# RWKV heads, a dense gated layer and routed experts: per-head products on quarters of TensorE, and a new order ahead of the dense stage

## The reference

```python
# 1: 4 sequences, 8 heads, 768 steps, 48 wide
for t in range(S):
    kt, vt, rt = k[:, :, t], v[:, :, t], r[:, :, t]
    cur = einsum('bhd,bhe->bhde', u[None] * kt, vt)
    y[:, :, t] = einsum('bhd,bhde->bhe', rt, state + cur)
    state = w[None, :, :, None] * state + einsum('bhd,bhe->bhde', kt, vt)
# 2: x (3072, 384), ff 1536
x = (silu(x @ w_gate) * (x @ w_val)) @ w_out
# 3: 8 experts, ff 1024, the best one per token
logits = x @ w_gate2;  e = argmax(logits);  gate = softmax(logits)[e]
out = gate * sigmoid(x @ w_output_gate)[e] * (relu(x @ w1[e]) @ w2[e])
```

## Time and profile before

| | us |
|---|---|
| Runs | 886.81, 887.0, 889.1 (median 887.0) |
| Profiled execution | 887.55 |
| its span | 885.7 |
| TensorE busy | 851.0 |
| VectorE busy | 570.2 |
| ScalarE, POOL busy | 316.5, 182.4 |
| First dense matmul starts | 44.65 |

### The profile page before, as it was taken

The page is one execution under the profiler, slowest core; times in us unless marked ns, Lnnn a source line. Parts: engine busy times, 40 slices in busy tenths (PEclk is TensorE's granted clock), DMA queues, the critical chain, the costliest instruction groups (busy, mean ns, idle before and its releaser), DMA issues.

```text
span 885.7 us, 15606 instructions
## 1 busy us (share of the span) xinstructions
PE 851.0 (96%) x5725; PEld 759.2 (86%) x5725; DVE 570.2 (64%) x1045; ACT 316.5 (36%) x503; POOL 182.4 (21%) x145
## 2 busy tenths in 40 slices
PE   5799999999999999999999999999699999999996
PEld 4688888888888888888888888899699999999995
DVE  8778756675568546543444446467778778977771
ACT  1233223111311131112211221356176766777661
POOL 4923202232123403140101001003112111011110
PEclk9999999999999999999999999999799999999999
DMA  9843420242024402340010002547397778766700
GB/s 380 285 162 132 132 105 13 83 153 83 0 64 128 135 1 65 100 130 1 11 45 36 1 1 80 208 180 238 144 415 258 260 278 302 263 237 252 286 17 19
DMA packets 35935, 125.79 MB, mean 142 GB/s; under 512 B 4044, under 2 KB 19328, under 8 KB 30256
## 3 DMA queue, kind: packets, MB, share of 16 engines
q1 hardware_dynamic: 31504, 108.20, 34.4%
q0 software_dynamic: 3520, 9.87, 2.9%
q10 hardware_dynamic: 864, 7.08, 2.2%
HBM read 107.32 MB, written 18.88 MB: 142 GB/s over the span
## 4 chain that ended last, share of the span: by engine, by line
PE 91%; DVE 3%; DMA 3%; issue 2%; POOL 1%; ACT 0%; POOLq 0%; DVEq 0%
PE bank L1525 33%; PE bank L1569 6%; PE bank L1571 6%; PE bank L1570 6%; PE bank L1622 4%; PE bank L1620 4%; PE bank L1621 4%; PE bank L1601 4%; PE bank L1602 3%; PE bank L1603 3%; PE bank L1598 3%; PE bank L1450 3%; PE bank L1470 2%; PE bank L1435 2%; PE bank L1462 2%
## 5 line engine op out<-in xcount | busy, mean ns | idle before, releaser
L1525 PE MATMUL bank<-X1H,WH 128*128 128x512 f32 x432 | 169.5, 392 | 4.2 <-DVE X1L L1040 4.2
L1525 PE MATMUL bank<-X1H,WL 128*128 128x512 f32 x432 | 168.9, 391 | 0.0
L1525 PE MATMUL bank<-X1L,WH 128*128 128x512 f32 x432 | 168.7, 390 | 0.0
L1186 DVE TENSOR_TENSOR TT<-bank,SG 128x512 f32<-128x512 f32 x72 | 49.7, 691 | 120.5 <-ACT SG L764 120.0
L764 ACT ACTIVATE SG<-bank 128x512 f32<-128x512 f32 x72 | 43.0, 598 | 234.6 <-PE bank L1525 229.9
L694 ACT ACTIVATE AH<-PP 128x512 fp32r<-128x512 f32 (+1 forms) x78 | 46.2, 599 | 162.3 <-DVE PP L1191 162.3
L1525 PEld LDWEIGHTS bank<-X1H,WH 128*128 128x128 f32 x432 | 81.5, 189 | 21.1 <-issue 4.3
L1525 PEld LDWEIGHTS bank<-X1H,WL 128*128 128x128 f32 x432 | 81.4, 188 | 17.1
L1194 DVE TENSOR_TENSOR AL<-PP,AH 128x512 fp32r<-128x512 f32 (+1 forms) x78 | 63.2, 817 | 50.9 <-ACT AH L694 49.4
L1525 PEld LDWEIGHTS bank<-X1L,WH 128*128 128x128 f32 x432 | 81.6, 189 | 16.7
L1569 PE MATMUL bank<-AH,WH 128*128 128x512 f32 (+1 forms) x234 | 91.0, 389 | 0.0
(11 more groups left out here) (225 smaller groups left out, 1859.6 us busy)
## 6 DMA issues: line engine op xcount, KB each, us to landing
W_EVEN<-w SPq DMA_DIRECT2D x20, 1536.0 KB, 9.1
W_ODD<-w SPq DMA_DIRECT2D x18, 1536.0 KB, 7.7
RK_IN<-unit_rk SPq DMA_DIRECT2D x18, 736.0 KB, 5.6
V_IN<-unit_v SPq DMA_DIRECT2D x18, 448.0 KB, 3.8
STG<-w_dense ACTq DMA_DIRECT2D x6, 1152.0 KB, 5.9
X<-mixed SPq DMA_DIRECT2D x6, 768.0 KB, 4.4
mixed<-YS SPq DMA_DIRECT2D x40, 96.0 KB, 2.0
XG_ODD<-store SPq DMA_DIRECT2D x9, 394.0 KB, 8.5
```

The lines of the kernel that those rows point to most:

```text
L1186: tt(TT[:, :], GATE_PS[:, :], SG[:, :], ALU.mult).then_inc(gate_free, 1)
L1525: last = mm(bank_[:, :], lhs[:, f, m, k * P:k * P + P], rhs[:, k, :], start=(x == 0), stop=(x == len(terms) - 1))
```

## The change

Key sums and the state's part of the outputs are made per head: SELU and ST lose the empty halves (64 and 48 columns in place of 112), and each head's product takes 48 rows and up to 64 columns on one quarter of the array. Heads are placed so that the row half and the column half of a head are chosen apart (class `Head`: x rows, g columns, s place among the keys). Products of the two row halves go to two banks: outputs to banks 5 and 6, key sums to 7 and 0, the gate's bank; units 0 to 5 keep one bank for their key sums and make them in two parts. `own_key` and `add_output` read two banks with two instructions each, state decay and state addition take one instruction in place of two. `scores` and the masked part keep their counts of products. Routing uses the gate's bank, except at its last time, and stands ahead of the unit's pieces.

In the head the decays come in a transfer of their own; SELU is one copy; TensorE turns the identity 30 times first; POOL starts behind the power tables; VectorE scales k and r of unit 4 too and takes all six slices of the first weights' low part; X1 is stored, loaded and split in four parts of 128 tokens; units 6 and 7 are loaded behind X1; outputs and state terms of unit 5 move into step 0 of block 0. The diff, cut:

```diff
+HEAD_AT = ((0, 1, 2, 3), (5, 4, 7, 6))
+HALF_COLS = PAIRS * P // 2
+class Head:
+    def __init__(self, h):
+        self.h, self.j, self.g = h, h // 2, h % 2
+        self.x = 0 if h in HEAD_AT[0] else 1
+        self.s = HEAD_AT[self.x].index(h)
+        self.rows = slice(64 * self.x, 64 * self.x + HD)
+        self.out = 64 * self.g
+        self.keys = slice(self.s * P, self.s * P + P)
+        self.cols = slice(self.j * P, self.j * P + P)
+BY_QUARTER = [Head(h) for h in (0, 5, 1, 4, 2, 7, 3, 6)]
...
+    SELU = place(a, "SELU", [PR, PAIRS, 64])
+    ST = place(a, "ST", [PR, BATCH, PAIRS, HD])
...
-                self.scores = bank[5], bank[6]
-                self.c_bank, self.y, self.u = bank[7], bank[5], bank[6]
+                self.scores = self.y = bank[5], bank[6]
+                self.c_banks, self.u = (bank[7], bank[0]), bank[7]
...
         def _(sp):
-            sp.dma_start(CST[:, :], consts).then_inc(consts_loaded, 16)
+            sp.dma_start(CST[:, C_W:C_ID], consts[:, C_W:C_ID]).then_inc(decays_loaded, 16)
+            sp.dma_start(CST[:, C_ID:C_ALL], consts[:, C_ID:C_ALL]).then_inc(consts_loaded, 16)
...
+            def load_x1_part(b):
+                sp.wait_ge(y_start_stored[b], 32)
+                sp.dma_start(X1[:, :, b * P:b * P + P], mixed_tiles[:, :, b * P:b * P + P]).then_inc(x1_part_loaded[b], 16)
             store_output(Unit(0, 0))
+            store_output(Unit(0, 1))
+            load_x1_part(0)
+            load_x1_part(1)
+            store_output(Unit(0, 2))
+            store_output(Unit(0, 3))
+            load_x1_part(2)
+            load_x1_part(3)
             load_unit(Unit(1, 2))
             load_unit(Unit(1, 3))
-            for b in range(1, BATCH):
-                store_output(Unit(0, b))
-            sp.wait_ge(y_start_stored, 32 * BATCH)
-            sp.dma_start(X1[:, :, :], mixed_tiles[:, :, 0:BLK]).then_inc(x1_loaded, 16)
...
         def _(pool):
+            pool.wait_ge(pow_turned, 1)
             scale_rk(u0)
             scale_rk(u1)
+            pool.wait_ge(r_start_scaled, 3)
             pool.wait_ge(tables_ready, 1)
...
-            first_low(0)
             scale_rk(u4)
-            scale_k(u4)
-            scale_r(u4)
             scale_rk(u5)
+            pool.wait_ge(r_start_scaled, 5)
             scale_k(u5)
             scale_r(u5)
             scale_kt(u4)
             scale_kt(u5)
-            first_low(1)
+            pool.wait_ge(x1_low, KT)
...
         def _(act):
+            for b in range(BATCH):
+                first_state(b)
+            x1_high_part(0)
+            x1_high_part(1)
             split_dense(0)
-            first_state(2)
-            first_state(3)
+            x1_high_part(2)
+            x1_high_part(3)
...
         def _(dve):
-            dve.wait_ge(consts_loaded, 16)
+            dve.wait_ge(decays_loaded, 16)
+            nc.vector.tensor_copy(SELU[:, :, :], ucol.unsqueeze(2).broadcast_to([PR, PAIRS, 64])).then_inc(select_ready, 1)
...
-                tt(u.ys, u.v[0:PR, I_VT:I_VV], u.c_bank[0:PR, :], ALU.mult).then_inc(c_used, 1)
+                for x in range(2):
+                    cols = slice(HALF_COLS * x, HALF_COLS * (x + 1))
+                    last = tt(u.ys[:, cols], u.v[0:PR, I_VT:I_VV][:, cols], u.c_banks[x][0:PR, cols], ALU.mult)
+                last.then_inc(c_used, 1)
...
-                    tt(old, old, WPOW[r:r + HD, :, 7:8].broadcast_to([HD, PAIRS, HD]), ALU.mult).then_inc(decayed, 1)
+                tt(ST[:, u.b, :, :], ST[:, u.b, :, :], WPOW[:, :, 7:8].broadcast_to([PR, PAIRS, HD]), ALU.mult)\
+                    .then_inc(decayed, 1)
...
+            mask_scores(u0)
+            dve.wait_ge(pow_turned, 2)
+            mask_scores(u1)
+            first_scales(u2)
+            own_key(u0)
+            add_output(u0)
+            own_key(u1)
+            add_output(u1)
+            first_scales(u3)
+            mask_scores(u2)
+            own_key(u2)
+            mask_scores(u3)
+            own_key(u3)
+            add_output(u2)
+            add_output(u3)
+            first_scales(u4)
+            dense_lows(0, (0,))
+            x1_low_part(0)
+            x1_low_part(1)
+            mask_scores(u4)
+            own_key(u4)
+            x1_low_part(2)
+            x1_low_part(3)
+            finish_unit(u4)
+            dense_lows(0, (1, 2))
+            mask_scores(u5)
+            own_key(u5)
...
         def _(pe):
+            def key_sums(u, quarters=BY_QUARTER):
...
-                for j in range(PAIRS):
-                    last = mm(u.c_bank[0:PR, j * P:j * P + P], SELU[:, j, :], u.rxk[:, j * P:j * P + P],
+                for a in quarters:
+                    width = HD if a.g else 64
+                    last = mm(u.c_banks[a.x][a.out:a.out + width, a.cols], SELU[a.rows, a.s, 0:width], u.rxk[a.rows, a.keys],
                               start=True, stop=True)
...
-                    for j in range(PAIRS):
-                        mm(u.y[0:PR, j * P:j * P + P], ST[:, u.b, j, :], u.rw[:, j * P:j * P + P],
-                           start=(j == 0), stop=False, skip_group_check=True)
+                    for a in BY_QUARTER:
+                        mm(u.y[a.x][a.out:a.out + HD, a.cols], ST[a.rows, u.b, a.s, :], u.rw[a.rows, a.keys],
+                           start=(a.j % 2 == 0), stop=False, skip_group_check=True)
...
+            for x in range(30):
+                nc.tensor.transpose(bank[2][:, 0:P], ident, ident)
+            scores(u0)
+            scores(u1)
...
             outputs(u4)
             state_terms(u4)
-            outputs(u5)
-            state_terms(u5)
+            key_sums(u5, STRAIGHT)
+            scores(u5)
+            key_sums(u5, CROSSED)
...
             def dense_block(n):
+                    if f % 2 == 1 and f // 2 < len(units):
+                        pe.wait_ge(c_used, units[f // 2].i + 1)
                     up(GATE_PS, 0, f, n).then_inc(gate_ready, 1)
                     need(pe, value_free, q)
                     up(VALUE_PS, 1, f, n).then_inc(value_ready, 1)
+                    if not first and f in (0, 1, 2, 3, 5):
+                        if f == 0:
+                            turn(n)
...
+                    if first and f == 0:
+                        outputs(u5)
+                        state_terms(u5)
                     if f // 2 < len(units):
                         u = units[f // 2]
                         if f % 2 == 0:
+                            pe.wait_ge(gate_free, q + 1)
                             key_sums(u)
                             scores(u)
```

More of the change, by code:

```diff
@@ L247, in __init__ @@
             self.odd = b % 2
+            self.behind = self.i - 1 if isinstance(c, int) and self.i == AHEAD else self.i
             self.start = isinstance(c, int) and self.i < AHEAD
@@ L1436, in key_sums @@
                               start=True, stop=True)
-                last.then_inc(c_ready, 1)
+                if quarters[-1].h == 6:
+                    last.then_inc(c_ready, 1)
+                else:
+                    last.then_inc(straight_sums, 1)
+            STRAIGHT = [a for a in BY_QUARTER if a.x == a.g]
+            CROSSED = [a for a in BY_QUARTER if a.x != a.g]
             def scores(u):
-                pe.wait_ge(k_start_scaled if u.first else k_scaled, u.i + 1)
-                pe.wait_ge(r_start_scaled if u.first else r_scaled, u.i + 1)
+                by_dve = u.start and u.i <= BATCH
+                pe.wait_ge(k_start_scaled if by_dve else k_scaled, u.i + 1)
+                pe.wait_ge(r_start_scaled if by_dve else r_scaled, u.i + 1)
@@ L1442, in scores @@
                 if u.start:
                     need(pe, masked, 2 * u.i - 2 if u.i >= 2 else 0)
+                    need(pe, y_added, BATCH if u.i == AHEAD - 1 else 0)
                 else:
-                    pe.wait_ge(y_added, u.i)
-                    pe.wait_ge(state_ready, min(u.i, UNITS - BATCH) if isinstance(u.i, int) else u.i)
-                for j in range(PAIRS):
-                    for half in range(2):
-                        r = 64 * half
-                        last = mm(u.scores[half][:, j * P:j * P + P], u.kw[r:r + HD, j * P:j * P + P],
-                                  u.rw[r:r + HD, j * P:j * P + P], start=True, stop=True)
-                        if j == PAIRS - 1:
+                    pe.wait_ge(y_added, u.behind)
@@ L1453, in scores @@
+                for s in range(PAIRS):
+                    for x in range(2):
+                        a = Head(HEAD_AT[x][s])
+                        last = mm(u.scores[x][:, a.keys], u.kw[a.rows, a.keys], u.rw[a.rows, a.keys], start=True, stop=True)
+                        if s == PAIRS - 1:
                             last.then_inc(scores_ready, 1)
@@ L1475, in state_terms @@
                 pe.wait_ge(kt_scaled, u.i + 1)
-                if u.start:
-                    need(pe, state_ready, min(u.i, BATCH))
-                for j in range(PAIRS):
```

(11 more changed lines are left out.)

317 lines of the change are left out of this document (151 added, 166 removed).

## The result

Four runs after: 878.01 to 880.20 us, median 879.37. Four before, shared with them: 886.81 to 889.1, median 887.99. The ratio is 0.9899 with an interval of 0.9879 to 0.9919: 8.6 us less, and the interval leaves no doubt that it is faster. The forecast of 876.0 was 3.4 us too low and its range held. The quarters brought about what was forecast for them; the new head brought almost nothing.

A forecast was written before the change was run, and what follows sets the result against it. TensorE, 91% of the chain, was taken as the bound. Terms -9.0 + 1.6 + 0.3 - 6.7 - 1.6 + 2.1 + 2.0 = -11.3 took the profiled 887.55 to 876.2, stated as 876.0 us, range 870 to 883.

The forecast's parts named there:

- (c): First step of blocks 1 to 4: TensorE stands still 0.4 us for own_key beside POOL's product, 1.6 us for four.
- (d): Block 5: turning logits and counting ranks in bank 0, with a wait behind each, costs 0.3 us.
- first dense matmul: End of the head: the first dense matmul starts near 37.9 instead of 44.65, 6.7 us less (36 to 41).
- first 18 dense matmuls at full clock: Start of the dense stage: 18 matmuls take 4.1 instead of 5.81 us, 1.6 less if TensorE comes busy.
- unit 5's outputs in block 0: Outputs and state terms of unit 5, moved from the head into block 0, add 2.1 us there.
- wait for own_key of unit 6: Block 0's first key sums: TensorE waits 2.0 us (0 to 3.5) while VectorE finishes unit 5, then own_key.
- rival B: Quarters help, head does not: u4's mask slips 4 to 5 us, dense at 43, TensorE cold; 882 us, chance 0.17.
- Four slots for eight, less two changes of division: Key sums and state part in dense blocks: 0.44 less 0.19 is 0.25 us per piece, 9.0 for 18 units.
- Rival D: Slower: quarters do not run four abreast, so 36 pieces cost 0.19 us more each; 892 us, chance 0.07.
- (b): Dense blocks: the next gate product waits until own_key has read both banks; 0.2 us slack left, so nothing.
- rival C: The gate's wait for own_key binds, 0.4 us in each of 14 steps, 5.6 in all; 881.5 us, chance 0.08.
- a dense low, which needs ScalarE's first_state(3), two X1 parts and a split, to 31.3: VectorE's head work after u4's scales at 29.5: this low part ends at 31.3, u4's mask at 33.5.

The follow-up runs named there:

- e8: Changed kernel with the dense blocks' key sums in two calls of two quarters each, scores between them: 894.19 us, ratio 1.0051.
- e7: Changed kernel with the later units' state_terms at 48 columns of weights again instead of 64 for the first half: 882.08 us, ratio 0.9912.
- e11: Changed kernel with 52 turns of the identity in TensorE's 6.0 us wait for unit 4's mask: 880.2 us, ratio 0.9915.
- e2: Changed kernel with the heads reordered so that the two of a quarter follow each other: 878.94 us, ratio 0.9901.
- e1: Changed kernel with unit 4's mask and own_key moved ahead of the first weights' low part and two of X1's: 878.51 us, ratio 0.9896.
- e4: e1 with X1 loaded in one transfer behind all four stores, its splits still in four parts: 876.6 us, ratio 0.9875.
- e5: e4 with ScalarE's weight split first, and VectorE's weight low parts and finish_unit(u4) ahead of X1's low parts: 877.72 us, ratio 0.9865.
- e6: e5 with a one-column sigmoid added on ScalarE to load the sigmoid's table early: 877.94 us, ratio 0.9862.
- e9: e6 with 18 turns of the identity, ten ahead of unit 4's scores and eight ahead of its outputs: 877.82 us, ratio 0.9876.
- e10: e9 and e7 together, the 18 turns plus state_terms of 48 columns: 877.04 us, ratio 0.987.
- e3: Changed kernel without the 30 turns of the identity at the start of TensorE's queue: 878.21 us, ratio 0.9884.

## Why the forecast was right, and where it was not

The total lies in the forecast's range; the quarters' mechanism was right, the head's was not, and part of the agreement is luck. By its own terms, on the profiled executions (-9.6; forecast -11.3):

| step | forecast | measured |
|---|---|---|
| key sums and state part, 18 units | -9.0 | -9.7 |
| state_terms, wider weights | none | +1.6 |
| (c) first steps of blocks 1 to 4 | +1.6 | 0 |
| (d) block 5 | +0.3 | +0.7 |
| first dense matmul | -6.7 | -1.85 |
| first 18 dense matmuls at full clock | -1.6 | -1.5 |
| unit 5's outputs in block 0 | +2.1 | +2.0 |
| wait for own_key of unit 6 | +2.0 | +1.1 |
| expert stage | 0 | -1.7 |

The measured terms add up to -9.35; 0.25 us has no term. The expert stage's 1.7 us are luck: the change does not touch it. If the medians hold the same 1.7 (only the profiled pair shows it), the change alone would stand at about 881: still in the range, but nearer to rival B's 882 than to the forecast's 876.0. By the forecast's own signs the head was wrong: the first dense matmul stood behind 41, and a wait of over 3 us (6.00) came ahead of it, B's sign.

- **Four slots for eight, less two changes of division.** Right: 0.27 us per piece against 0.25. The price of a change, read from pieces that divide the array in another way, carried over to quarters: 0.09 ahead of the piece, and 0.60 - 4 x 0.11 = 0.16 in it, against 0.96 - 0.88 = 0.08 before, so 0.17 more where 0.19 was taken. (The working for it was rough: 1.09 - 0.88 is 0.21 and not 0.1, but it holds a change on either side of the scores.) The Trainium skill ("TensorEngine Tiling (Array Packing)", Key Properties) has a drain at each switch of the tiling mode; the trace agrees that there is a cost and gives its size. Rival D is ruled out, and e8 shows what it would have been like: with two abreast in the key sums alone the change ends slower than before.
- **state_terms at nothing.** Wrong, and the forecast does not name it: I counted products, and the counts are the same, but not the columns of the weights. The diff's ST goes from 48 to 64 columns for half of the heads, and 16 short records with 48 moving columns cost 0.55 in place of 0.46; e7 takes it back. 1.6 us over 18 units.
- **(c), 0.4 us in each first step.** Wrong on the cautious side. I let own_key run beside POOL's product, at double time. It does not: it takes 0.75 in two instructions at 142.93, and TensorE's gate starts at 143.82 without a wait. (b) is 0 as forecast, so rival C falls.
- **(d).** The wait of 0.3 is there, ahead of the gate that follows turn_logits, and that gate's first matmul comes 0.15 later still. The next two steps are 0.17 and 0.11 longer than before; what causes that was not tried.
- **The head up to X1.** The first scaling is at 7.79 (forecast 7.8), the last add_output of block 0 ends at 26.47 (forecast 28.2, so better than thought).
- **"a dense low, which needs ScalarE's first_state(3), two X1 parts and a split, to 31.3".** This is the step that failed. The forecast priced the way to X1's last part (a store's landing, a load's landing), and that was nearly right: 2.3 and 2.5 us, the last part there at 35.3 for 34.1. It put at nothing the landings of units 0 and 1, on which the first two parts depend and for which SyncE's queue stands still. They took 7.2 to 10.9 us with the queues full, so those parts were asked for at 27.88 and 28.5, ScalarE reached the split at 31.50, and VectorE, done with u4's scales at 28.46 (forecast 29.5), stood 3.90 us in the middle of its list. The mask of u4 ended at 36.17 for 33.5: 2.7 us. The other 2.3 of the 4.9 us between 37.9 and 42.80 are TensorE's: u4's and u5's pieces took 42.80 - 36.31 = 6.49 us for 4.2, at half clock, and at the full one dense starts at 40.57 (e11). (The forecast's own terms add up to 37.7.)
- **Rival B** has the mechanism and the place, the split behind X1 and u4's mask behind the split, dense at 43. It had the mask slip by 4 to 5 us, which it did not, and the cold stretch return in the dense stage; it stood ahead of it.
- **The smaller wait of unit 6 (1.1 for 2.0)** follows from that: TensorE came later, VectorE did not. The other moves of the head (the power tables, POOL's start, the loads behind X1) were not tried one by one.

Had the X1 parts come as assumed, would the 6.7 us have been there? The runs that start the dense stage earlier say no (start in us; the last column is step 1, from the second gate to the next):

| | first dense | second gate | block 1 | step 1 |
|---|---|---|---|---|
| changed kernel | 42.80 | 52.04 | 136.56 | 8.53 |
| e2, same head | 43.01 | 51.98 | 136.57 | 8.52 |
| e7, same head | 43.65 | 53.10 | 137.26 | 8.42 |
| e1 | 37.54 | 51.23 | 137.31 | 10.08 |
| e4 | 38.99 | 50.17 | 134.69 | 8.53 |
| e5 | 39.72 | 50.52 | 135.06 | 8.54 |
| e6 | 39.51 | 49.79 | 134.27 | 8.48 |
| e9 | 37.33 | 49.11 | 136.17 | 11.06 |
| e10 | 38.22 | 49.59 | 135.37 | 10.05 |
| e11 | 40.57 | 52.13 | 137.98 | 9.85 |

The gain of 2.2 to 5.5 us at the first milestone is 2.9 at best at the second and 2.3 at best at block 1. The rest turns into a wait of 0.4 to 4 us for own_key, behind VectorE's work or, in e9 and e11, behind the store of unit 4; and where that wait is 2.4 us or more (e1, e9, e10, e11), step 1 runs in part at half clock and takes 1.3 to 2.5 us more. My 2.0 us for the wait was an estimate for 37.9; at 37.5, e1 shows 1.55 + 3.97, and 1.55 more in step 1. e4, e5 and e6 keep 1.5 to 2.3 us at block 1, more than e2 and e7 differ by with one and the same head (0.7). In the total that is at the edge of what these runs can tell: by median e4, e5, e6 and e10 are 1.4 to 2.8 us below the changed kernel, on different chips, and the expert stage's wait alone varies by more. What stays open is why that wait varies (5.5 to 9.4 us); it stands behind the scatter of the routed tokens, whose landing took 7.03 us before and 5.37 after, and no run was made on it.

## What to carry to other kernels

When short products fill only part of the array, count slots, not flops: eight 48-row products on four quarters took the place of four on the full array for 0.27 us less a piece, but the columns of the stationary side have a price too, and with key sums only two abreast the sign turned (e8). A gain at the start of a stage is not a gain until the next place where the engines meet: put the milestone behind the first handovers that other engines owe and behind the half clock that a wait there brings (here the start of block 1), and ask what they still have to do by then. And price every landing that an order waits for, the first ones too, from a row with the queues as full as they will be: an order in which one queue waits for such landings between its stores delays the very data it wants early.

## What the runs showed of the hardware that was not expected

- Order does not matter among the quarters: alternating or paired, 16 records take 0.60 us (e2), and 8 on two quarters take 0.58 (e8).
- Stationary width costs for short products: 16 records of 48 moving columns take 0.55 us with 64 columns of weights and 0.46 with 48 (e7).
- Turning an fp32 identity raises the clock. After 30 turns in 4.90 us, scores ran at 1.16 us; without them at 2.08 (e3). 18 and 52 turns kept the full level (2.4 GHz) through the stretch ahead of the dense stage in e9 and e11; in e10 the same 18 did not (0.68 from 35 to 40). The Trainium skill ("TensorE: Matmul & The Clock Gate", Part 4) has it that the clock does not go to its full level for TensorE's transpose mode, which does not count as busy in the same way; these traces do not agree for fp32 turns of the identity (a turn leaves one record where an fp32 product leaves two; the trace does not name the mode).
- Two idle stretches, of 1.27 and 0.92 us, were followed by 13 us at the half level (1.2 GHz) with hardly a pause in e5 (31 to 44.6 us), and by 3 us of it in e1, with the same two ahead (1.26 and 0.92). The rows ahead of both are alike, so a forecast of the clock from one trace is not safe.
- In the head the full level came back, and was lost again at the next wait for VectorE: 2.44 us (e10), 3.5 (e11), 3.70 (e9) and 3.97 (e1) at the second gate were each followed by a clock of 0.55 to 0.66 over 50 to 55 us; 1.13 (the changed kernel), 0.8 (e4) and 0.4 (e5, e6) were not.
- The stores of units 0 and 1 landed after 7.2 to 10.9 us behind queued loads, those of units 2 and 3, from 28.95 on, after 2.3 to 2.7; over all units the median landing of such a store on the page is 2.1.
